# First layers as seven block products (one level of Strassen's scheme)

## What is computed

```python
def _moe_ref(x, w_gate, w1, w2):            # x: 1152 x 512, 8 experts
    P = np.exp(logits - logits.max())       # logits = x @ w_gate
    for _ in range(8):                      # Sinkhorn rounds
        P /= P.sum(1, keepdims=True) + 1e-09
        P /= P.sum(0, keepdims=True) + 1e-09
        P *= N / E
    for e in range(E):
        h = np.maximum(x @ w1[e], 0.0)      # 512 -> 1024
        out += P[:, e:e + 1] * (h @ w2[e])  # 1024 -> 512
def _moe2_ref(x, w_a, w_b, w_out):          # 512 -> 1536, 1536 -> 512
    return (x @ w_a) * (x @ w_b) @ w_out
```

## Time and profile before

| | us |
|---|---|
| median of 3 runs | 1137.43 |
| lowest, highest | 1137.15, 1137.85 |
| the profiled execution's own time | 1137.25 |
| its span, first to last instruction | 1135.3 |
| TensorE's granted clock, mean | 1.000 (2.4 GHz) |

### The profile page before, as it was taken

How to read it: one execution, slowest core, us unless ns; L and a number is a source line. 1 busy time by engine, 2 the same in 40 slices (tenths; PEclk the granted TensorE clock), 3 DMA queues, 4 the chain that set the end, 5 groups by cost and what they waited for, 6 DMA issues and landing times.

```text
span 1135.3 us, 15451 instructions
## 1 busy us (share of the span) xinstructions
PE 1129.2 (99%) x6210; PEld 1023.7 (90%) x6210; DVE 403.7 (36%) x785; ACT 293.9 (26%) x603; POOL 51.2 (5%) x63
## 2 busy tenths in 40 slices
PE   9999999999999999999999999999999999999998
PEld 7778988999899899989989998998999899999997
DVE  7774443322241332224133222413322332433322
ACT  6885202212030221203122120312212131222210
POOL 1362300000000000000000000000000000000000
PEclk9999999999999999999999999999999999999999
DMA  9942202110120211012011101202100020110001
GB/s 202 220 112 86 74 1 56 57 38 11 64 74 0 57 54 37 18 55 74 0 64 49 35 18 55 74 0 74 47 28 10 28 75 1 56 56 21 18 29 55
DMA packets 52537, 59.14 MB, mean 52 GB/s; under 512 B 31600, under 2 KB 31600, under 8 KB 52496
## 3 DMA queue, kind: packets, MB, share of 16 engines
q1 hardware_dynamic: 51296, 58.27, 18.1%
q10 hardware_dynamic: 1200, 0.30, 0.1%
HBM read 56.15 MB, written 2.40 MB: 52 GB/s over the span
## 4 chain that ended last, share of the span: by engine, by line
PE 98%; SPq 1%; DMA 0%; DVE 0%; issue 0%; ACT 0%
PE bank L1205 16%; PE bank L1207 16%; PE bank L1206 16%; PE bank L1334 14%; PE bank L1336 14%; PE bank L1335 14%; PE bank L1153 2%; PE bank L1190 2%; PE bank L1084 1%; PE bank L1273 1%; PE bank L1124 0%; SPq L329 0%; PE bank L1042 0%; DMA nat<-in_k 0%; PE bank L1346 0%; PE bank L1165 0%
## 5 line engine op out<-in xcount | busy, mean ns | idle before, releaser
L1205 PE MATMUL bank<-xh,w1h 128*128 128x384 f32 x1056 | 354.2, 335 | 0.0
L1207 PE MATMUL bank<-xh,w1l 128*128 128x384 f32 x1056 | 353.0, 334 | 0.0
L1206 PE MATMUL bank<-xl,w1h 128*128 128x384 f32 x1056 | 352.9, 334 | 0.0
L1334 PE MATMUL bank<-w2h,hh 128*128 128x512 f32 x684 | 267.1, 390 | 0.0
L1336 PE MATMUL bank<-w2h,hl 128*128 128x512 f32 x684 | 266.3, 389 | 0.0
L1335 PE MATMUL bank<-w2l,hh 128*128 128x512 f32 x684 | 266.2, 389 | 0.0
L584 ACT ACTIVATE hh<-bank 128x384 fp32r<-128x384 f32 x192 | 94.5, 492 | 612.8 <-PE bank L1207 612.8
L1205 PEld LDWEIGHTS bank<-xh,w1h 128*128 128x128 f32 x1056 | 198.2, 188 | 1.1 <-issue 0.2
L1206 PEld LDWEIGHTS bank<-xl,w1h 128*128 128x128 f32 x1056 | 198.3, 188 | 0.7
L1207 PEld LDWEIGHTS bank<-xh,w1l 128*128 128x128 f32 x1056 | 198.2, 188 | 0.0
L830 DVE SCALAR_TENSOR_TENSOR hl<-bank,hh 128x384 fp32r<-128x384 f32 x192 | 106.9, 557 | 248.5 <-ACT hh L584 248.5
(11 more groups left out here) (116 smaller groups left out, 563.1 us busy)
## 6 DMA issues: line engine op xcount, KB each, us to landing
stage<-in_moe_w SPq DMA_DIRECT2D x64, 512.0 KB, 3.6
bias<-cum_dram SPq DMA_DIRECT2D x14, 256.0 KB, 4.0
stage<-in_moe_w_a SPq DMA_DIRECT2D x12, 256.0 KB, 2.6
stage<-in_moe_w_b SPq DMA_DIRECT2D x12, 256.0 KB, 2.9
stage<-in_moe_w_out SPq DMA_DIRECT2D x12, 256.0 KB, 2.6
bias_tail<-cum_dram SPq DMA_DIRECT2D x16, 144.0 KB, 4.4
nat<-in_q SPq DMA_DIRECT2D x16, 128.0 KB, 3.8
vt<-in_v SPq DMA_DIRECT2D x16, 128.0 KB, 4.0
```

Of the source, the lines that this page charges most:

```text
L1205: pe.matmul(o, w1h[:, c, col:col + PART], high, start=(c == 0), stop=False)
L1206: pe.matmul(o, w1h[:, c, col:col + PART], low, start=False, stop=False)
L1207: ins = pe.matmul(o, w1l[:, c, col:col + PART], high, start=False, stop=(c == KC - 1))
L1334: pe.matmul(o, hh[:, n % 2, f, at], w2h[:, f, :], start=(f == 0), stop=False)
```

## The change

The first layer of a pair of feature chunks is made by seven block products rather than eight. With the weights cut into 2 by 2 blocks (input feature half by chunk: `W10, W00, W01, W11`; the two chunks of a pair are f and f + 4 of an expert, or a chunk of w_a and of w_b in the multiplying layers) and x cut into 2 by 2 blocks (input feature half by batch), sums of blocks are made once: four of weights per pair (`mix`, GpSimd, into `mixed`) and four of x (T1 to T4: `sum_t` on VectorE, split into `th`, `tl`; T4 takes the place of a block of x). Each product accumulates 2 input chunks times 3 terms, 6 matmuls, of 256 columns (tokens 0 to 255 of a batch) or 320 (the rest); the two widths are two "sets" of a pair. VectorE combines the products with additions from PSUM into SBUF (`kept`), where intermediate values stand unsplit; the rectified values are split from there.

Intermediate values are made in two halves: an expert makes 2 pairs (4 sets), then the second layer over their 4 chunks for all 9 tiles, and the same again; the addition to `acc` happens 16 times a tile, not 8. For the first half, tiles are copied unweighted into `acc` during the Sinkhorn rounds, and weighted afterwards (`weigh`). The gate has w_gate's high and low parts side by side in one operand (`wg`) and needs two terms, not three. Weight splits of the next pairs are made during the second layer. In the last expert, x blocks and T sums are made from the transposed tiles (`low_x2`, `high_x2`, `low_x2_sums`). SBUF's layout changes for all of this; first-layer banks are four, second-layer banks three (two for the first half).

The core of the diff:

```diff
-        def layer1(e, n, f, w, view, halfway=None):
-            for c in range(KC):
-                high, low = view(xh4, n, c), view(xl4, n, c)
-                pe.matmul(o, w1h[:, c, col:col + PART], high, start=(c == 0), stop=False)
-                pe.matmul(o, w1h[:, c, col:col + PART], low, start=False, stop=False)
-                ins = pe.matmul(o, w1l[:, c, col:col + PART], high, start=False, stop=(c == KC - 1))
+        READ_BY = {1: u3_done, 2: u4_done, 6: c10_done, 7: c01_done, 5: one_kept, 4: c00_done, 3: u2_done}
+        def product(n, i, nth, place, s, first=False):
+            bank = product_bank(nth, n, first)[:, 0:width(s)]
+            if not first:
+                pe.wait_ge(READ_BY[n], i if n in (1, 2, 6, 7) else i + 1)
+            for c in range(2):
+                high, low = w1h[place][:, LEFT[n], c, :], w1l[place][:, LEFT[n], c, :]
+                pe.matmul(bank, high, right(n, False, c, s), start=(c == 0), stop=False)
+                pe.matmul(bank, high, right(n, True, c, s), start=False, stop=False)
+                ins = pe.matmul(bank, low, right(n, False, c, s), start=False, stop=(c == 1))
+            ins.then_inc(product_mm[n], 1)
+    PRODUCTS = (1, 2, 6, 7, 5, 4, 3)
...
+        def mix(unit, place, loads):                      # GpSimd
+            put(0, w[:, W10, :, :], w[:, W11, :, :], ALU.add)
+            put(2, w[:, W00, :, :], w[:, W10, :, :], ALU.subtract)
+            put(1, to[:, 0, :, :], w[:, W00, :, :], ALU.subtract)
+            put(3, w[:, W01, :, :], to[:, 1, :, :], ALU.subtract)
...
+        def half_of_sets(e, h):                           # VectorE, a set
+                    add_c00(i, nth, s)                    # product 2 + kept product 1
+                add_u2(i, nth, s, early)                  # product 6 + kept product 1
+                add_u3(i, nth, s, early)                  # product 7 + u2
+                add_c11(i, nth, s, early)                 # product 5 + u3
+                add_u4(i, nth, s, early)                  # product 5 + u2
+                add_c10(i, nth, s, early)                 # product 4 + u3
+                low_hidden(i, 2 * h + m, s, 1)
+                add_c01(i, nth, s, early)                 # product 3 + u4
+                low_hidden(i, 2 * h + m, s, 0)
+                for c in {0: (0, 1), 1: (2,), 2: (3,)}.get(n, ()):
+                    low_w2(2 * e + h, c)
+                if second and n >= 2:
+                    for tile in range(0, 5) if n == 2 else range(5, NT):
+                        weigh(tile)
...
+        def half_of_sets(e, h):                           # ScalarE, a set
+                    keep_one(i, nth, s)
+                    high_hidden(i, nth, 2 * h + m, s, 0, 0)
+                high_hidden(i, nth, 2 * h + m, s, 1, 1)
+                high_hidden(i, nth, 2 * h + m, s, 1, 0)
+                high_hidden(i, nth, 2 * h + m, s, 0, 1)   # halves 0 also rectify in place
...
+        def half_of_sets(e, h):                           # GpSimd
+                    low_hidden(8 * e + nth, nth, 2 * h + m, s, 0)
+                low_hidden(8 * e + nth, nth, 2 * h + m, s, 1)
+                if n % 2 == 0:
+                    mix(4 * e + 2 * h + 2 + m, m, 2 * e + h + 2)
...
+        def layer2(half, tile, halfway=None):             # 12 matmuls of 512
+            elif isinstance(half, int) and half == 1 and tile == 0:
+                pe.wait_ge(acc_weighed, NT)
+            for nth, place in enumerate((0, 2, 1, 3)):
+                pe.matmul(bank, hh[:, place, at], w2h[:, place, :], start=(nth == 0), stop=False)
+                pe.matmul(bank, hh[:, place, at], w2l[:, place, :], start=False, stop=False)
+                ins = pe.matmul(bank, hl[:, 3 - place, at], w2h[:, place, :], start=False, stop=(nth == 3))
...
+        product(5, 0, 0, 0, 0, True)                      # after attention, TensorE
+        pe.wait_ge(x_lo, 2 * PAIRS)
+        gate(1, 0, range(2, KC))
+        gate(1, 1, range(2, KC))
...
+                pe.wait_ge(t_lo, T_NTH[2, 1])             # first set of expert 0
+                make_first(6, 0, c00_done, 1)
+                pe.wait_ge(t_lo, T_NTH[3, 1])
+                make_first(7, 0, one_kept, 2)
+                transpose_gate()
+                pe.wait_ge(t_lo, T_NTH[4, 1])
+                make_first(4, 0, c00_done, 2)
+                make_first(3, 0, u4_done, 1)
...
+        def multiply(j, n, s, b):                         # GpSimd, multiplying layers
+            pool.tensor_tensor(one[:, 0:width(s)], one[:, 0:width(s)], two[:, 0:width(s)], ALU.mult).then_inc(ab_done, 1)
...
+                    if g == 0 and n == 0 and p == 7:      # TensorE, after the experts
+                        x2_read(NT - 2)
```

More of the change, by code:

```diff
@@ L1404, in result2 @@
[L1404 to L1423 removed]
+        half_of_sets(E - 1, 0)
```

1245 lines of the change are left out of this document (778 added, 467 removed).

## The result

The changed kernel takes 1117.1 us in the median of four runs (1115.6 to 1118.5), the kernel before 1137.4 (1137.15 to 1137.85): a ratio of 0.9821, 95% interval 0.9804 to 0.9838, so 1.8% faster. The prediction was 1102 with a range of 1086 to 1126. The sign and the range hold; the likeliest value is 15 us too low, a quarter of the 58 us of TensorE time that the change takes away, and the measured time lies above the narrower forecast of 1094 to 1110.

What follows compares the result with a forecast made beforehand. The rate of matmuls on TensorE was taken as the bound. 58 us saved and 23 given back at the seams turned a span of 1135.3 us into 1100.1, timed as 1102 us; range 1086 to 1126.

Steps and rivals of the forecast that it cites:

- narrower forecast: Whole kernel: a time of 1094 to 1110 us around the likeliest 1102, given a 53% chance.
- Matmuls removed: First layer and gate: fewer matmul columns, starts 0.120 and 0.147 us apart at 256 and 320 columns, 58 us less TensorE time.
- Rival 3: Product matmuls: the weight load holds 256-column ones at 0.133 us, 22 us more, 1124 us; chance 6%.
- rival 5: Product matmuls: the 13 ns beyond columns/2.4 fall away at narrower widths, 48 us less, 1054 us; chance 2%.
- No stall in steady sets: Steady sets: VectorE's additions meet every bank deadline, smallest slack 1.36 us (u4), so no stall.
- Rivals 2 and 4: Rival 2: port waits in most sets, 1120 us, 14%. Rival 4: VectorE waits out GpSimd's whole mixing run, 1168 us, 10%.
- The port: Steady sets: VectorE waits for one GpSimd operation of 0.74 or 0.87 us, under the slack; at most 0.2 a set.
- Attention's end: End of attention: T sums and low parts on VectorE beside GpSimd make TensorE wait 10 us, range 3 to 12.
- Sinkhorn: Copying of tiles 3 to 8: a round plus copy and w1 low part exceeds a tile's time, 2 us.
- The weighing: Before the second half's first tile: nine VectorE passes of 512 elements hold TensorE for 4 us (2.5 to 5).
- x2: After the last tile: transposes wait 1.3 us, then product 5 waits 4.9 for ScalarE; together 6 us (4 to 9).
- Multiplying layers: Third and fourth weight units split between sets, 2 us of VectorE ahead of a c01 addition with 1.7: 1 us.

Runs made afterwards that it cites:

- slack_2: Changed kernel plus two more VectorE operations of 512 columns in each of the loop's 48 sets, results unread: 1127.6 us, one run.
- gp_late: Changed kernel with GpSimd's splitting of the second unit's blocks moved from the middle of attention's end to behind VectorE's last T matrix: 1116.1 us.
- filler: Changed kernel plus unread 512-column matmuls on TensorE ahead of the five waits (17, 8, 16, 17 and 8 of them): 1111.1 us.
- expert0: Changed kernel with the first expert's weighing moved out of the sets to behind each second-layer tile, Sinkhorn's last column sums three products later: 1106.4 us.
- x2_order: Changed kernel with the multiplying layers' first products, ScalarE's copy of product 1 and three VectorE additions moved ahead of last-tile work: 1114.2 us.
- ab_split: Changed kernel with, in the multiplying layers, the first part of the next unit's low values taken ahead of the C10 addition: 1116.4 us.
- seams2: Changed kernel with expert0, x2_order and revised gp_late2 and ab_split edits: logits ahead of low parts, no set with both layers' low parts: 1097.0 us.
- gp_late2: gp_late with VectorE's four low parts of the second layer's first weights taken in sets 1 and 2 instead of 0 to 2: 1116.9 us.
- mix_twice: Changed kernel plus four more unread mixing-kind additions on GpSimd with every unit of the loop, 96 in all: 1130.9 us, one run.

## Why the prediction held, and where it was off

By its own steps, in us, the sum against the profiled run:

| stretch | predicted | measured | difference |
|---|---|---|---|
| to the end of expert 0 | 95.7 + 125.3 = 221.0 | 227.2 | +6.2 |
| loop | 562.6 | 562.8 | +0.2 |
| last expert, x2, multiplying layers | 104.0 + 208.9 = 312.9 | 99.6 + 221.0 = 320.6 | +7.7 |
| from there to the end | 3.6 | 3.6 | 0 |
| span | 1100.1 | 1114.2 | +14.1 |

- **Matmuls removed: right.** 0.120 and 0.147 us at 256 and 320 columns, the loop at 562.8. The estimate (columns + 32)/2.4 ns holds at two more widths. Rival 3 (0.133) and rival 5 (13 ns less) fall by the same rows. The Trainium skill's N/2.4 + 2.5 ns (TensorE: Matmul & The Clock Gate, section Back-to-back issue gap) would be 0.109 and 0.136; the page gives it for a matmul taken by itself, and the trace disagrees here as it did at 384. The prediction's "24 matmuls" for a pair and three token blocks is a slip (24 are one block's); its sum has the right 72.
- **No stall in steady sets: right**, with the size of the slack shown by slack_2. Rivals 2 and 4 fall: no wait in the loop's 48 sets and 24 mixings. But the measured 1117 is nearer to rival 2's 1120 than to the likeliest 1102 or its band up to 1110, and the range reaches above 1110 only for rivals 2 and 3, neither of which came true. That the range held is in part luck.
- **The port: right in kind, and its place was missed.** In the loop VectorE's low parts of 320 columns take 0.64 us in the mean against 0.48 alone, 48 of them, so 0.16 us each in turns, inside the slack. At attention's end the turns are worth 3.6 us on three operations (gp_late). The Trainium skill (SBUF — State Buffer, section Who interferes with whom) states the exclusion; 6.31 us in the changed kernel against 2.76 in gp_late agrees. What the prediction did not ask is which queue stands next in line for the same port when GpSimd's work moves.
- **Attention's end: the sum right, its parts less so**, 10 predicted, 9.7 measured as waits. The walk gave 3 us side by side and 7 for the turns on the port. By starts the changed kernel's waits from 97 to 125 us come to 8.4 us; with GpSimd's splitting away (gp_late) the same places still have 6.3, before the new wait at 126. So this splitting is worth 2 us of waiting at these places, and most of the rest is there without it. Sinkhorn: 2 predicted, 1.3.
- **The weighing: mis-sized**, 4 predicted and 7.5 measured. The 3.7 to 3.9 for the first tile is the predicted mechanism at its size. Added to it are 1.65 us for a product in set 3, whose c00 stood behind the five weighings of set 2 (the prediction let the slack take them; beside GpSimd they took 0.8 us each, not 0.57), and 2.0 for the last column sums, which the prediction did not walk through: TensorE asks for them after the third product of the set behind the round that feeds them.
- **x2: 6 predicted, 7.8 measured**, by the two waits that were named (1.6 and 4.1) and the third weight unit's low part (2.0), which had been put under the multiplying layers at less than one.
- **Multiplying layers: 1 predicted, 3.5 measured.** The step gave two low parts 2 us; they are 2.2 alone, 2.7 beside GpSimd, and a second-layer low part of 0.68 stands in the same row. The slack of 1.7 was set against one of the three.
- **The clock: left out altogether, 8.4 us.** With waits of at most 1.3 us the kernel before held 1.00 through the stages, and the prediction carried that over to a kernel for which it forecast waits of 4 to 10 us. The Trainium skill (TensorE: Matmul & The Clock Gate, section What's actually happening) says that half rate is the default and activity releases it; the trace before could not show its price, but this was the term to bound. It is the largest single error, a term put at nothing, and filler shows it: the stretches go when TensorE has something to do in place of the waits.

The stalls come to 29.8 us where 23 were predicted (+6.8) and the clock to 8.4; what is left, the stages' own matmuls and small things, is about 1 us less than predicted (1.7 less in expert 0, 0.8 more elsewhere): 14. By the prediction's own sign of being wrong (the seams far from 23), the seams with the clock behind them are 38. The profiled run's 1116.0 is 1.8 above its span, and the median of four is 1.1 higher again, at granted clocks of 0.991, 0.991, 0.988 and 0.988.

Of the four changes of order that follow from this, one gave what its waits promised (expert0), one half of it (x2_order), and two nothing that can be told from zero (gp_late, ab_split), because VectorE's operations met GpSimd's at another place. Together, and with seams2's further moves, they give 20 us.

## What to carry to other kernels

A trade of TensorE time for VectorE time is settled in the steady loop by a walk through one set with its bank deadlines, and that walk can be right to 0.2 us, as it was here; what is given back stands at the seams, where one-time work is queued among the sets. Put the seam's long operations one to a set and on the far side of whatever TensorE asks for next, and look before moving one which other engine it will then share the port with. Where waits of several microseconds are forecast in a kernel that had none, put a price on the clock behind each of them.

## What the runs showed of the chip that was not expected

- After a wait of 1.8 to 4.1 us TensorE ran at a granted 0.50 for 3 to 5 us in the changed kernel and lost 1.4 to 2.2 us beyond the wait. The price of one wait is not fixed: behind the weighing, with the same 3.7 us ahead, it was 1.5 us there and 2.7 to 2.9 in gp_late, x2_order and ab_split. Twelve waits of 1.3 us and twelve of 0.8 us in otherwise full loops left it at 1.00, while in seams2 three waits of 1.2 us and less, close together, had a stretch at 0.50 behind them. What decides is open.
- The cost differs between runs of one kernel, and with it the time: seams2 took 1095.8 us at a mean granted clock of 1.000 and 1098.7 at 0.996; gp_late2 1112.8 at 0.994 and 1118.3 at 0.986. The kernel before, without such waits, stayed within 0.7 us beside the changed kernel and between 1137.2 and 1139.1 beside the experiments, its longest runs at a mean of 0.998; so the clock can fall somewhere in it too.
- Even a wait that leaves the clock alone costs one or two starts of 0.1 us more behind it: 1.65 us for 1.3 to 1.4 of waiting.
- A tensor-scalar operation from SBUF to SBUF on VectorE, one tensor input, takes longer beside GpSimd too: two of 512 columns took 1.70 us beside GpSimd's mixing, 1.03 with one low part of GpSimd beside them and 0.75 with GpSimd idle (slack_2). GpSimd is held up in turn: mixing operations of 0.74 us took 0.99 to 1.07 beside VectorE's low parts (mix_twice).
